# Linear-attention recurrence in steps of 64 tokens in place of 128, between dense layers on one core

## What is computed

```python
for t in range(S):
    cur = np.einsum('bhd,bhe->bhde', u[None] * kt, vt)
    y[:, :, t] = np.einsum('bhd,bhde->bhe', rt, state + cur)
    state = w[None, :, :, None] * state + np.einsum('bhd,bhe->bhde', kt, vt)
...
h = np.maximum(x @ w_in, 0.0)
    conv_out += conv_w[k][None, None, :] * hp[:, k:k + S, :]
return (h * gate @ w_out).astype(np.float32)
...
xn = (x - mu) / np.sqrt(var + 1e-06) * g_ln
ch = np.maximum(xn @ w_ch1, 0.0) @ w_ch2
return (x + ch).astype(np.float32)
```

## Time and profile before

| | us |
|---|---|
| median of 3 runs (622.5 to 625.73) | 623.82 |
| the profiled execution | 625.42 |
| its span, first to last instruction | 623.4 |
| PE busy | 612.7 (98%) |
| DVE busy | 412.4 (66%) |
| ACT busy | 287.6 (46%) |
| POOL busy | 135.6 (22%) |

### The profile page before, as it was taken

How to read it: one execution, slowest core, us unless ns; L and a number is a source line. 1 busy time by engine, 2 the same in 40 slices (tenths; PEclk the granted TensorE clock), 3 DMA queues, 4 the chain that set the end, 5 groups by cost and what they waited for, 6 DMA issues and landing times.

```text
span 623.4 us, 11031 instructions
## 1 busy us (share of the span) xinstructions
PE 612.7 (98%) x4440; PEld 556.8 (89%) x4440; DVE 412.4 (66%) x662; ACT 287.6 (46%) x576; POOL 135.6 (22%) x142
## 2 busy tenths in 40 slices
PE   8989999999999999999999999999999999999997
PEld 4678889999999999999999999999999999999996
DVE  5899978587563886455875638864558755386344
ACT  3878544475323563324653225643246532465330
POOL 3820152202241102241022421023410222000110
PEclk9999999999999999999999999999999999999999
DMA  8945120310202222021102032220211000010001
GB/s 269 295 169 220 30 89 1 111 40 30 68 1 80 101 69 68 1 68 44 46 24 69 1 89 92 68 69 0 70 43 42 28 2 1 1 44 1 0 1 43
DMA packets 11761, 38.79 MB, mean 62 GB/s; under 512 B 1728, under 2 KB 4672, under 8 KB 11712
## 3 DMA queue, kind: packets, MB, share of 16 engines
q1 hardware_dynamic: 11712, 38.11, 18.8%
HBM read 33.38 MB, written 4.72 MB: 61 GB/s over the span
## 4 chain that ended last, share of the span: by engine, by line
PE 92%; DVE 3%; DMA 1%; issue 1%; ACT 1%; SPq 0%; POOL 0%; DVEq 0%; POOLq 0%
PE acc L419 14%; PE acc L421 13%; PE hid L419 13%; PE acc L420 13%; PE hid L420 13%; PE hid L421 13%; PE att_ps L436 4%; PE att_ps L476 3%; PE att_ps L471 2%; PE att_ps L483 1%; DMA const<-consts 1%; PE att_ps L450 1%; DVE w_lo L853 1%; PE att_ps L581 0%; PE att_ps L580 0%
## 5 line engine op out<-in xcount | busy, mean ns | idle before, releaser
L419 PE MATMUL acc<-ring_hi,w_hi 128*128 128x440 f32 (+1 forms) x420 | 152.4, 363 | 0.6 <-DVE w_lo L853 0.6
L421 PE MATMUL acc<-ring_hi,w_lo 128*128 128x440 f32 (+1 forms) x420 | 151.8, 361 | 0.0
L420 PE MATMUL acc<-ring_lo,w_hi 128*128 128x440 f32 (+1 forms) x420 | 151.4, 361 | 0.0
L707 ACT ACTIVATE ring_hi<-hid 128x440 fp32r<-128x440 f32 (+1 forms) x84 | 44.4, 533 | 112.8 <-PE hid L421 112.8
L968 DVE SCALAR_TENSOR_TENSOR ring_lo<-hid,ring_hi 128x440 fp32r<-128x440 f32 (+1 forms) x84 | 50.8, 610 | 68.4 <-ACT ring_hi L707 68.4
L419 PE MATMUL hid<-x_hi,w_hi 128*128 128x440 f32 (+1 forms) x252 | 94.1, 373 | 0.1
L420 PE MATMUL hid<-x_lo,w_hi 128*128 128x440 f32 (+1 forms) x252 | 91.6, 363 | 0.0
L421 PE MATMUL hid<-x_hi,w_lo 128*128 128x440 f32 (+1 forms) x252 | 91.2, 362 | 0.0
L419 PEld LDWEIGHTS acc<-ring_hi,w_hi 128*128 128x128 f32 x420 | 78.9, 188 | 6.1 <-DVE w_lo L853 1.0
L421 PEld LDWEIGHTS acc<-ring_hi,w_lo 128*128 128x128 f32 x420 | 78.8, 188 | 5.0
L420 PEld LDWEIGHTS acc<-ring_lo,w_hi 128*128 128x128 f32 x420 | 78.8, 188 | 4.9
(11 more groups left out here) (148 smaller groups left out, 968.2 us busy)
## 6 DMA issues: line engine op xcount, KB each, us to landing
raw_n<-rkv_n SPq DMA_DIRECT2D x22, 576.0 KB, 4.3
rk<-rk_t SPq DMA_DIRECT2D x22, 448.0 KB, 3.6
w_raw<-weights SPq DMA_DIRECT2D x10, 768.0 KB, 7.9
out<-x SPq DMA_DIRECT2D x18, 220.0 KB, 2.1
first_raw_n<-rkv_n SPq DMA_DIRECT2D x2, 576.0 KB, 13.6
first_rk<-rk_t SPq DMA_DIRECT2D x2, 448.0 KB, 10.2
out<-x SPq DMA_DIRECT2D x3, 218.0 KB, 2.1
const<-consts SPq DMA_DIRECT2D x1, 192.0 KB, 7.9
```

The costliest lines, as they stand in the source:

```text
L419: mm(ps, lh, rh, start=start, stop=False)
L420: mm(ps, lh, rl, start=False, stop=False)
L421: return mm(ps, ll, rh, start=False, stop=stop)
L707: nc.scalar.activation(ring_hi[:, tile % RING, 0:n], hid[f % 2][:, 0:n], ACT.Relu).then_inc(act_hi, 1)
```

## The change

From chunk 6 on (the second to the fourth batch, 18 of the 24 chunks) a chunk is two steps of 64 tokens. The first six chunks stay as they are.
- `scores`: the scores between the chunk's two halves are no longer made, the state carries them. 16 matmuls of 48 rows, 64 weight columns and 64 moving columns, each in one quarter of the array (a half of its rows and a half of its columns), four quarters in turn.
- `kv`: 16 matmuls of 64 rows, 48 weight columns and 48 moving columns, again in four quarters in turn, into the free part of the scores' two PSUM banks, which are now one tensor, `sc_ps`. It stands directly behind `scores`, and the last chunk of a batch has it too (`NOT_LAST`), for its halfway state.
- `masked` is one DVE operation over 8 x 64 scores, into `att_half`, and waits for `kv` too. `mid` on DVE and `halfway` on ACT make and decay the state between the halves, by w to the 64th; three state buffers in turn (`state_of`).
- `y`: the state products keep their form (112 rows, 64 weight columns), now with another state for either half, and for the second half of a batch's first chunk too. The four `att` products become 64 rows, 64 weight columns, 48 moving columns: they lie in two quarters of the array, on its diagonal.
- Once, in unit 0: the powers of w for half chunks (`half_powers` on ACT, `half_by_token` on PE: four transposes, `half_powkt` on ACT) and a load of a mask of 64 x 64.
- All tables are written anew around this.

```diff
-    ("mm1", 0), ("mm1", 1), ("mm1", 2), ("scores", 0), ("mm1", 3), ("mm1", 4), ("mm1", 5), ("mm2", 0), ("kv", 0),
-    ("y", 0), ("scores", 1), ("xt", 0), ("mm1", 6), ("mm1", 7), ("mm2", 1), ("mm2", 2), ("mm2", 3), ("mm2", 4),
...
+    ("mm1", 0), ("mm1", 1), ("mm1", 2), ("mm1", 3), ("scores", 0), ("kv", 0), ("mm1", 4), ("mm1", 5), ("mm2", 0),
+    ("mm1", 6), ("mm1", 7), ("y", 0), ("scores", 1), ("kv", 1), ("xt", 0), ("mm2", 1), ("mm2", 2), ("mm2", 3),
...
-OF_STATE = {"kv", "state", "kd", "decay"}
+NOT_LAST = {"state", "halfway"}
...
-                if m < CHUNKS and not (kind in OF_STATE and m % CH == CH - 1):
+                if m < CHUNKS and not (kind in NOT_LAST and m % CH == CH - 1):
...
-def states_made(m):
-    return (CH - 1) * (m // CH) + min(m % CH + 1, CH - 1)
-def decays_made(m):
-    return (CH - 2) * (m // CH) + min(m % CH, CH - 2)
+def states_made(m, half=1):
+    if m < CH:
+        return min(m + 1, CH - 1)
+    return CH - 1 + (2 * CH - 1) * (m // CH - 1) + min(2 * (m % CH) + half + 1, 2 * CH - 1)
+def decays_made(m, half=0):
+    if m < CH:
+        return min(m, CH - 2)
+    return CH - 2 + (2 * CH - 2) * (m // CH - 1) + 2 * (m % CH) + half
+def kvs_made(m):
+    return min(m + 1, CH - 1) if m < CH else m
...
+        att_half = at("att_half", [P, H, HALF], f32, att_place)
...
+        state_of = lambda m, half=0: state[m % 2 if m < CH else (2 * m + half) % 3]
...
+        hid_pair, sc_pair = pair("hid"), pair("sc_ps")
...
+        att_ps = [sc_pair[:, i, :] for i in range(2)] + [bank("att_ps")]
...
+                if m >= CH:
+                    for hp in range(NP):
+                        for q in range(2):
+                            rows = slice(64 * q, 64 * q + D)
+                            for t in halves:
+                                last = mm(sc_pair[t, q, hp * HALF:(hp + 1) * HALF], rk_of(m)[rows, 1, hp, t],
+                                          rk_of(m)[rows, 0, hp, t], start=True, stop=True)
+                    last.then_inc(pe_sc, 1)
+                    return
...
-                pe.wait_ge(pool_kd, states_made(m))
+                pe.wait_ge(pool_kd, kvs_made(m))
...
+                if m >= CH:
+                    for hp in range(NP):
+                        for q in range(2):
+                            cols = slice((2 * hp + q) * D, (2 * hp + q + 1) * D)
+                            for half, t in enumerate(halves):
+                                last = mm(sc_pair[64 * q:64 * q + D, half, KV_AT + hp * D:KV_AT + (hp + 1) * D],
+                                          raw_n_of(m)[t, 1, cols], v_of(m)[t, cols], start=True, stop=True)
+                    last.then_inc(pe_kv, 1)
+                    return
...
-                if c:
+                if m >= CH:
+                    state_there(pe, m, 0)
+                elif c:
...
+                for hp in range(NP) if m >= CH else ():
+                    for half, t in enumerate(halves):
+                        if c or half:
+                            mm(y_ps[t, hp * 2 * D:(hp + 1) * 2 * D], rk_of(m)[0:ROWS, 0, hp, t],
+                               state_of(m, half)[0:ROWS, hp, :], start=True, stop=False)
+                    for q in range(2):
+                        cols = slice((2 * hp + q) * D, (2 * hp + q + 1) * D)
+                        for half, t in enumerate(halves):
+                            alone = not c and not half
+                            last = mm(y_ps[t, cols], att_half[t, NP * q + hp, :], v_of(m)[t, cols],
+                                      start=alone, stop=alone or q == 1)
+                for hp in range(NP) if m < CH else ():
                     for t in halves if c else ():
                         mm(y_ps[t, hp * 2 * D:(hp + 1) * 2 * D], rk_of(m)[0:ROWS, 0, hp, t],
-                           state[m % 2][0:ROWS, hp, :], start=True, stop=False)
+                           state_of(m)[0:ROWS, hp, :], start=True, stop=False)
...
+                pe.wait_ge(act_half, 2)
+                pe.wait_ge(act_xh, m + 1)
+                pe.wait_ge(dve_xl, m + 1)
+                for hp in range(NP):
+                    last = nc.tensor.transpose(att_ps[2][:, hp * P:(hp + 1) * P], tab[:, hp, :], ident)
+                last.then_inc(pe_tab, 1)
...
+            def decay(m, half=0):
...
-                state_there(act, m - 1)
+                w_over = w_far if m < CH else w_half
+                old, behind = state_of(m, half), state_of(m + 1) if m < CH else state_of(m, half + 1)
+                state_there(act, *(m, 0) if half else (m - 1,))
...
-                    last = copy(behind[0:ROWS, hp, :], old[0:ROWS, hp, :], scale=w_far[0:ROWS, hp:hp + 1])
+                    last = copy(behind[0:ROWS, hp, :], old[0:ROWS, hp, :], scale=w_over[0:ROWS, hp:hp + 1])
...
+            def halfway(m):
+                decay(m, 1)
+            def half_powers():
+                for hp in range(NP):
+                    last = copy(tab[:, hp, :].rearrange("p (j t) -> p j t", j=2),
+                                powk[:, hp, 32:96].unsqueeze(1).to_broadcast([P, 2, HALF]), scale=w_half[:, hp:hp + 1])
+                last.then_inc(act_half, 1)
...
+                if m >= CH:
+                    x = rk_of(m)[0:ROWS, :, :, :].rearrange("p a h (j t) -> p (a h) j t", j=2)
+                    by = powrk[0:ROWS, :, :, 32:96].rearrange("p a h t -> p (a h) t").unsqueeze(2).to_broadcast(
+                        [ROWS, 2 * NP, 2, HALF])
+                    tt(x, x, by, ALU.mult).then_inc(dve_rk, 1)
+                    return
...
+                if m >= CH:
+                    if m == CH:
+                        dve.wait_ge(ld_half, 16)
+                    dve.wait_ge(pe_kv, kvs_made(m))
+                    tt(att_half[:, :, :].rearrange("p (q h) t -> p q h t", q=2),
+                       sc_pair[:, :, 0:KV_AT].rearrange("p q (h t) -> p q h t", h=NP),
+                       mask_half.unsqueeze(1).unsqueeze(1).to_broadcast([P, 2, NP, HALF]), ALU.mult).then_inc(dve_mask, 2)
+                    return
...
+            def new_state(m, half=1):
+                first = m % CH == 0 and half == 0
+                dve.wait_ge(pe_kv, kvs_made(m))
+                if first:
+                    dve.wait_ge(pe_y, m)
                 else:
-                    dve.wait_ge(pe_y, m)
-                behind = state[(m + 1) % 2]
+                    dve.wait_ge(act_dec, decays_made(m, half) if m >= CH else decays_made(m))
+                if m < CH:
+                    behind, new_ps = state_of(m + 1), banks_of(m)[3][:, 0:NP * D]
+                else:
+                    behind, new_ps = state_of(m, half + 1), sc_pair[:, half, KV_AT:KV_AT + NP * D]
...
+            def mid_state(m):
+                new_state(m, 0)
```

More of the change, by code:

```diff
@@ new lines @@
+    ("scores", 0), ("warm", 1), ("by_token",), ("scores", 1), ("filler", 1), ("kv", 0), ("scores", 2),
[9 rows of a table added]
+PE_PLAN = [
[7 rows of a table added]
+ACT_FIRST = [
+    ("powers",), ("powkt",), ("cv", 0), ("state",), ("decay", 1), ("gains",), ("cv", 1), ("xh", 0), ("decay", 2),
+    ("cv", 2), ("decay", 3), ("xh", 1), ("cv", 3), ("w_hi", 0), ("xh", 2), ("decay", 4), ("xh", 3),
+    ("half_powers",), ("mean", 0), ("w_hi", 1), ("relu", 0), ("relu", 1), ("relu", 2), ("relu", 3), ("table",),
+    ("sig", 0), ("sig", 1), ("sig", 2), ("hi", 0), ("w_hi", 2), ("hi", 1), ("hi", 2), ("relu", 4), ("sig", 3),
+    ("relu", 5), ("w_hi", 3), ("hi", 3), ("sig", 4), ("xh", 4), ("relu", 6), ("sig", 5), ("weigh", 1), ("hi", 4),
+    ("relu", 7), ("sig", 6), ("hi", 5), ("w_hi", 4), ("half_powkt",), ("sig", 7), ("hi", 6), ("hi", 7),
+    ("weigh", 2), ("x2_hi", 0), ("w_hi", 5), ("x2_hi", 1), ("x2_hi", 2), ("fhi", 0), ("mean", 1), ("fhi", 1),
+    ("x2", 0), ("w_hi", 6), ("fhi", 2), ("x2", 1), ("x2", 2), ("xh", 5), ("mean", 2), ("fhi", 3), ("sum_hi", 0),
+    ("square", 0), ("w_hi", 7), ("fhi", 4), ("fhi", 5), ("w_hi", 8), ("halfway", 6), ("fhi", 6), ("square", 1),
+    ("square", 2), ("sum_hi", 1), ("fhi", 7), ("fhi", 8), ("w_hi", 9), ("fhi", 9), ("fhi", 10), ("root",),
+    ("fhi", 11), ("xh", 6)]
@@ L151 @@
+    ("small", "g"), ("load_t", 2), ("load_n", 1), ("load_n", 2), ("load_t", 3), ("load_w", "c1_0"), ("load_n", 3),
+    ("loads", 4), ("load_w", "in0"), ("loads", 5), ("load_w", "in1"), ("small", "cw"), ("load_w", "out0"),
+    ("load_w", "out1"), ("load_w", "c1_1"), ("small", "half"), ("loads", 6), ("load_w", "c1_2"),
+    ("load_w", "c2_0"), ("loads", 7), ("load_w", "c2_1"), ("load_w", "c2_2"), ("loads", 8), ("results", 0),
+    ("results", 1), ("results", 2)]
 SP_PLAN = [
@@ L270, in bank @@
             return ctx.enter_context(nc.psum_tensor(name, [P, 512], f32))
-        hid = [bank(f"hid{i}") for i in range(2)]
+        pair = lambda name: ctx.enter_context(nc.psum_tensor(name, [P, 2, 512], f32))
+        hid_pair, sc_pair = pair("hid"), pair("sc_ps")
+        hid = [hid_pair[:, i, :] for i in range(2)]
         acc = [bank(f"acc{i}") for i in range(KT)]
```

(17 more changed lines are left out.)

144 lines of the change are left out of this document (69 added, 75 removed), and 28 rows, old and new, of tables (PE_FIRST, PE_PLAN).

## The result

| | before | after |
|---|---|---|
| median (us) | 623.59 (622.5 to 625.73) | 635.39 (634.72 to 636.12) |
| profiled execution | 625.42 | 634.72 |
| its span | 623.4 | 632.8 |

The ratio is 1.0194 (95% interval 1.0174 to 1.0215): slower by 1.9%. The forecast was 634.3 us, between 628.5 and 645.5.

What follows compares the result with a forecast made beforehand. PE, busy 98% of the span at its full clock, was taken as the bound, so its own instructions count in full. The terms summed to +10.5 us on 623.8, giving 634.3 us, range 628.5 to 645.5.

Steps and rivals of the forecast that it cites:

- Changes of form within `y`: Switching the part of the array used between state and `att` products, 126 times at 0.137 us: +17.3 us.
- rival A: Changes of form inside `y` are free, as both kinds use half the columns: -6.8 us, 617.0 us; chance 12%.
- `scores`, -8.6: `scores` as 32 records in four quarters at once takes 0.51 us, saving 0.48, 18 times: -8.6 us.
- Rival B: The quarters don't work four at once; `scores` takes 0.87 us, `kv` 0.72: sum +21.6, 645.4 us; chance 10%.
- `kv`, 0.36: `kv` in four quarters takes 0.36 us, unchanged for 15 chunks; three last chunks of batches gain one: +1.1 us.
- First chunks' state products: The `y` of a batch's first chunk gets four state products of one half, 3 x 4 x 0.17: +2.1 us.
- the 12 fewer changes elsewhere: Changes of form outside `y` fall from 86 to 74, at 0.15 us each: -1.8 us.
- terms 1 to 5: On PE: changes within `y` +17.3, `scores` -8.6, `kv` +1.1, first chunks' state products +2.1, other changes of form -1.8 us.
- DVE, ACT, POOL, SP at nothing: Changed work on the engines besides PE makes PE wait nowhere, dense matmuls covering the halfway state: 0 us.
- C: Some `y` also waits for its mask or halfway state behind DVE: +3 to +8, 637 to 642 us; chance 8%.
- The start, -1 to +2: Start tables are written anew; PE stands for 6.7 of the first 60 us: -1 to +2 us.
- D: A change inside `y` costs half, 0.06 to 0.08 us: -7 to -10 on the sum, 624 to 628 us; 6%.

Runs made afterwards that it cites:

- run 1: The changed kernel plus one bf16 matmul of zeros over the result bank ahead of each changed `y`, product order kept (seven changes of form): 639.41 us.
- run 2: As run 1, but two pairs' state products, then these pairs' `att` products, twice: three changes of form within a `y` in place of seven; 628.59 us.
- run 3: As run 1, but all state products of a `y` first, then all `att` products: one change of form in place of seven; 623.45 us.
- run 7: Run 6 with each state product cut into one per head, alternating with that head's `att` products, no change of form within `y`: 632.5 us.
- run 5: The changed kernel with each state product cut into one per head, alternating with that head's `att` products: fifteen changes of form within a `y`; 672.38 us.
- run 4: The kernel before, with a zero matmul ahead of each `y` that has state products, and these grouped ahead of all `att` products: 629.13 us.
- run 6: The changed kernel with 128 rows in the `att` products again, no change of form within `y`, and DVE's mask in two instructions: 627.67 us.
- run 9: Run 3's order without the zero matmul, first products opening the sums: 621.3 us; a second kernel, this with DVE's mask in two instructions: 629.42 us.
- run 8: The changed kernel with `scores` and `kv` reordered: eight records in one quarter, then the next quarter, in place of quarters in turn; 658.85 us.

## Why the prediction held, point by point

1. *Changes of form within `y`, +17.3.* Right in its cause, and near in its size. 0.10 us of standing and 0.035 to 0.042 of an unhidden weight load, 0.137 together, is what the rows after show as well; the traces of runs 1 to 3 give 0.141 a change, 17.8 us for 126, their medians 0.148 and 18.6, and run 7 against run 5 gives 0.135. Runs 1 to 4 and 7 exclude rival A: the price belongs to the pair of forms, not to the order. By the rule that I quoted from the Trainium skill, "TensorEngine Tiling (Array Packing)", Tiling Modes, Key Properties, the term was 17.3; the trace agrees with it also for the pair that was missing, where only the rows' split differs.
2. *`scores`, -8.6.* 0.52 us instead of 0.99, 0.47 saved 18 times: -8.5. Right. Rival B needed 0.87.
3. *`kv`, 0.36.* 0.47 less the usual 0.09 to 0.10 of standing ahead of dense is 0.37. Right; 32 records in 0.37 us lie 12 ns apart, half of the 22.5 that B took for a floor. The Trainium skill, "TensorE: Matmul & The Clock Gate", section "Wait — 56ns, not 53.3ns?", has about 25 ns as the least distance from start to start: for records in different quarters the trace doesn't agree.
4. *First chunks' state products, the 12 fewer changes elsewhere, the tables of unit 0: +2.1, -1.8, +0.4.* No run took them apart. The first of them is 2.0 by its own product, 12 x 0.17; in chunk 6's `y`, which has the state products of one half only, a pair takes 0.67 us, as much as where both halves have them, so one half's products cost what I put on them. All blocks of the recurrence from chunk 6 on, each less the usual 0.20, add up to 72.48 us in place of 61.93, so +10.5, where terms 1 to 5 were +10.1. The other 0.7 of the +11.2 between the first dense matmul and the last lies in the dense work and in unit 0; 0.24 of it are waits between 60 and 540 us.
5. *DVE, ACT, POOL, SP at nothing.* Right: 0.27 us of waits between 60 and 540 us, against C, and DVE's busy time is 412.5 us where it was 412.4. How thin that cover is I didn't see: 0.69 us more of DVE a chunk, and PE waits 7 us (runs 6 and 9). I had called DVE "even" and named 45 dense matmuls between `kv` and `y` as the cover; the waits that came were not at `y` but at `raw_n`, which DVE makes, and at `ring_hi` and `conv_sb`, which ACT makes; run 9 added work to DVE alone, so DVE delayed these as well.
6. *The start, -1 to +2.* 1.8 us earlier in the profiled pair, outside of what I gave; against the medians there is nothing of it.
7. *The total.* The medians differ by 11.8, 1.3 more than the sum; before's own median came out 0.2 lower beside the changed kernel than in the runs I started from. That is the 1.1 us between 634.3 and 635.39. Of the 11.8, 10.5 are in the recurrence's blocks and 0.7 in the rest up to the last dense matmul. 0.6 lie outside, where the profiles differ by more than that whatever the kernel: the first dense matmul starts between 31.3 and 33.1 us. So the mechanism was right, and that the total is so close has some luck in it.

D, half the price, falls with 0.14 a change.

## What to carry to other kernels

Quarters of the array halved the time of `scores` (0.99 to 0.52 us), with neighbours in different quarters, but each change of form between neighbours costs about 0.14 us, as much as several of the products; so count the changes in PE's order before the products, and group products by form. A bank's sums need not be opened one by one: opened once for either half, they took all state products and then all `att` products, without a clearing product (run 9, 621.3 us). When PE is the bound at 98% and the next engine is at 65%, another 2% on that engine can still cost more than 1%, at places that have nothing to do with the edit.

## What the runs showed of the hardware that I had not expected

- The clock. A `y` of 16 groups of small products with a change of form between each takes 4 us, and the granted clock went to 0.50 at eight of 18 of them (run 5). With as many groups and no change of form, 1.9 us long, it never did (run 7), nor with seven changes in 2.5 us (the changed kernel).
- Four quarters run at once with records 12 to 16 ns apart (0.37 and 0.52 us for 32), if neighbours in the order lie in different quarters. With eight in one quarter behind one another, `scores` takes some 1.3 us (313.68 to the last of its records at 315.00), where one after another would be 1.73 and four at once 0.52 (run 8).
- By the trace PE starts records out of the program's order where they lie in different quarters, by a few at a time: in run 8 the first three of `kv`, each ahead of one of the last three of `scores`, and in run 3 two of `scores` (309.60) ahead of the last two of `att` (309.65).
- A DVE instruction on 64 partitions takes as long as on 128 (the mask of 512 elements a partition: 687 ns both), so cutting it in two doubles it. The line of run 6:

```profile
L970 DVE TENSOR_TENSOR att<-sc_ps,const 64x512 f32<-64x512 f32 x36 | 24.7, 687 | 0.9
```

and that of the changed kernel:

```profile
L969 DVE TENSOR_TENSOR att_half<-sc_ps,const 128x512 f32<-128x512 f32 x18 | 12.4, 687 | 0.3
```
